# Scores of the next tile first in TensorE's step, their copy early in ScalarE's, and GpSimd's low parts of the weights one step later

## The reference, cut to what matters

```python
# B, H, S, D = 2, 8, 576, 64; N = 1152 tokens of 512
scores = (q @ k.T) / sqrt(D)                       # 576 x 576 for each of 16 heads
kth = np.partition(scores, -32, axis=-1)[..., -32] # the 32nd largest of each row
scores = np.where(scores >= kth, scores, -1e9)
attn = softmax(scores)                             # exp(s - max) / (sum + 1e-9)
x = (attn @ v)                                     # 1152 x 512 after the heads are joined
h = x @ w_in                                       # 512 -> 2048
x = (h * sigmoid(h)) @ w_out                       # 2048 -> 512
P = exp(x @ w_gate - max), then 8 rounds of dividing by row sums and column sums
out = sum over 8 experts e of P[:, e] * (relu(x @ w1[e]) @ w2[e])   # 512 -> 1024 -> 512
```

## Time and profile before

| | us |
|---|---|
| median of three runs | 1318.68 |
| lowest and highest | 1318.45, 1321.45 |
| the profiled execution, its own time | 1318.84 |
| its span, first to last instruction | 1317.0 |
| TensorE busy | 1266.2 (96%) |
| VectorE busy | 655.0 (50%) |
| ScalarE busy | 457.2 (35%) |
| GpSimd busy | 365.8 (28%) |

### The profile page before, as it was taken

One profiled execution on the slowest core, in us unless ns is written; L12 is line 12 of the kernel. 1 busy time (PEld: TensorE's weight loads), 2 busy tenths in 40 slices (PEclk: granted clock), 3 DMA queues, 4 the chain that ended last, 5 costly groups with the idle time before them and its releaser, 6 DMA issues.

```text
span 1317.0 us, 21366 instructions
## 1 busy us (share of the span) xinstructions
PE 1266.2 (96%) x8109; PEld 1121.8 (85%) x8109; DVE 655.0 (50%) x1557; ACT 457.2 (35%) x960; POOL 365.8 (28%) x319
## 2 busy tenths in 40 slices
PE   6888999999999999999999999999999999999999
PEld 5677787887787898898898898898898998998997
DVE  6889999999999326422222222222222222222222
ACT  3666766767667323021121121121120220220210
POOL 2665434434444322031131131130230230330300
PEclk9999999999999999999999999999999999999999
DMA  5863746636536543120120120120220210210001
GB/s 139 290 213 122 270 154 226 219 97 222 197 126 237 218 193 95 32 64 19 47 64 13 52 64 0 63 64 0 64 64 0 64 60 3 64 49 15 0 0 72
DMA packets 72929, 130.14 MB, mean 99 GB/s; under 512 B 42016, under 2 KB 42016, under 8 KB 63648
## 3 DMA queue, kind: packets, MB, share of 16 engines
q1 hardware_dynamic: 72864, 129.27, 28.9%
HBM read 110.12 MB, written 19.14 MB: 98 GB/s over the span
## 4 chain that ended last, share of the span: by engine, by line
PE 78%; DVE 12%; POOL 5%; ACT 3%; issue 2%; DMA 0%; SPq 0%; ACTq 0%
PE banks L408 24%; PE banks L410 24%; PE banks L409 24%; DVE stats L861 5%; DVE rest L872 4%; PE banks L476 2%; POOL probs L1108 2%; POOL wd_lo L1086 2%; PE banks L443 2%; POOL wu_lo L1086 1%; PE banks L452 1%; DVE g_f L926 1%; PE banks L469 1%; ACT scores L684 1%; ACT wu_hi L760 1%
## 5 line engine op out<-in xcount | busy, mean ns | idle before, releaser
L821 ACT ACTIVATE h_hi<-banks 128x384 fp32r<-128x384 f32 x192 | 94.4, 492 | 624.8 <-PE banks L410 624.8
L408 PE MATMUL banks<-x_lo,wu_hi 128*128 128x384 f32 x768 | 257.2, 335 | 0.0
L410 PE MATMUL banks<-x_hi,wu_hi 128*128 128x384 f32 x768 | 256.8, 334 | 0.0
L409 PE MATMUL banks<-x_hi,wu_lo 128*128 128x384 f32 x768 | 256.8, 334 | 0.0
L1086 POOL TENSOR_TENSOR wu_lo<-wu_raw,wu_hi 128x512 fp32r<-128x512 f32 x76 | 95.9, 1299 | 559.4 <-ACT wu_hi L760 552.2
L987 DVE SCALAR_TENSOR_TENSOR h_lo<-banks,h_hi 128x384 fp32r<-128x384 f32 x192 | 106.8, 557 | 281.7 <-ACT h_hi L821 281.7
L1029 DVE SCALAR_TENSOR_TENSOR y_acc<-banks,plan_e,y_acc 128x512 f32<-128x512 f32 x135 | 101.3, 751 | 272.3 <-PE banks L410 272.3
L408 PE MATMUL banks<-wd_lo,h_hi 128*128 128x512 f32 x576 | 227.9, 396 | 0.0
L410 PE MATMUL banks<-wd_hi,h_hi 128*128 128x512 f32 x576 | 227.8, 396 | 0.0
L409 PE MATMUL banks<-wd_hi,h_lo 128*128 128x512 f32 x576 | 227.8, 396 | 0.0
L861 DVE MAX8 stats<-rest 128x8 f32<-128x576 f32 x216 | 156.1, 750 | 0.7
(11 more groups left out here) (103 smaller groups left out, 1810.2 us busy)
## 6 DMA issues: line engine op xcount, KB each, us to landing
wu_raw<-in_moe_w_dram SPq DMA_DIRECT2D x32, 512.0 KB, 3.7
wd_raw<-in_moe_w_dram SPq DMA_DIRECT2D x32, 512.0 KB, 3.7
wu_hi<-kept_up_hi SPq DMA_DIRECT2D x14, 1024.0 KB, 5.5
wu_lo<-kept_up_lo SPq DMA_DIRECT2D x14, 1024.0 KB, 8.5
wd_hi<-kept_down_hi SPq DMA_DIRECT2D x14, 1024.0 KB, 6.1
wd_lo<-kept_down_lo SPq DMA_DIRECT2D x14, 1024.0 KB, 8.5
q_nat<-in_q_dram SPq DMA_DIRECT2D x64, 72.0 KB, 2.2
wu_raw<-in_moe_w_in_dram SPq DMA_DIRECT2D x8, 512.0 KB, 4.6
```

The source lines that it names most:

```text
L408: pe.matmul(to, a_hi, b_lo, start=first, stop=False)
L409: pe.matmul(to, a_lo, b_hi, start=False, stop=False)
L410: return pe.matmul(to, a_hi, b_hi, start=False, stop=last)
L821: act.activation(h_hi[:, f, CH * c:CH * (c + 1)], ps_up[:, at % UBANKS, 0:CH], ACT.Relu).then_inc(h_hi_done, 1)
```

## The change

On TensorE `scores_of(step + 1)` becomes the first thing of the step, ahead of the first slice and of `weigh_values`. On ScalarE `copy_scores(step + 1)` moves from behind `copy_output` to right behind `copy_pT`, ahead of `g_high`, the first slice's tanh and `exp_scores`. On GpSimd the low parts of the weight pieces of a step are formed in the next step, right behind `lower_scores`. SyncE's loads of the next unit move one step later with them.

```diff
@@ SyncE
-                if split_at(step - 1):
-                    stream, n = split_at(step - 1)
-                    load_split(stream, n + 1, 0)
                 if split_at(step - 2):
                     stream, n = split_at(step - 2)
+                    load_split(stream, n + 1, 0)
+                if split_at(step - 3):
+                    stream, n = split_at(step - 3)
                     load_split(stream, n + 1, 1)
                     if n < SLOTS:
                         keep_unit(stream, n)
@@
-            load_split("down", UQ + 1, 1)
+            for half in range(2):
+                load_split("down", UQ + 1, half)
@@ TensorE
             for step in STEPS:
+                if step + 1 < ALL:
+                    scores_of(step + 1)
                 silu_slice(slice_at(step, 0))
                 if step < NT + FIRST_SLICE:
                     keep_clock(ps_m[:, 1, 0:P], 4)
                 if 0 <= step - 3 < ALL:
                     weigh_values(step - 3)
-                if step + 1 < ALL:
-                    scores_of(step + 1)
@@ ScalarE
                 if 0 <= step - 3 < ALL:
                     copy_pT(step - 3)
+                if step + 1 < ALL:
+                    copy_scores(step + 1)
                 g_high(slice_at(step - 1, 0))
@@
-                if step + 1 < ALL:
-                    copy_scores(step + 1)
                 split_pieces(pieces_at(step, 0))
@@ GpSimd
                     lower_scores(step - 2)
+                if step <= ALL:
+                    split_pieces(pieces_at(step - 1, 0))
+                    split_pieces(pieces_at(step - 1, 1))
@@
-                if step < ALL:
-                    split_pieces(pieces_at(step, 0))
-                    split_pieces(pieces_at(step, 1))
```

## The result

The changed kernel takes 1326.49 us, the median of six runs (1325.42 to 1332.27), against 1319.27 for the kernel before in the same comparison. The ratio is 1.0059, interval 1.0040 to 1.0078: slower by 7 us. I had forecast 1316.4 and a range up to 1321.5.

What follows compares the result with a forecast made beforehand. It took a ring of GpSimd, lower_scores and ScalarE to bound steps 4 to 18, and TensorE and VectorE in turns steps 23 to 71. The terms -10.4 + 8.1 = -2.3 us gave 1316.5, by the median 1316.4; range 1309.5 to 1321.5.

Steps and rivals of the forecast that it cites:

- The ring of low parts: Tiles 4 to 18: GpSimd's low parts, lower_scores and ScalarE's high part wait on each other, 6.00 us a step.
- The gain by filled waits for the transposed tile: Steps without a first slice: scores fill TensorE's 0.78 us wait, so 0.69 us goes away behind the values.
- tiles 4 to 18, -10.4 forecast: With low parts a step later, steps fall from 6.00 us to VectorE's 5.24; 10.4 us gained, bounds 5 to 11.1.
- four filler matmuls about 0.5: Tiles 4 to 18: time in us put down for TensorE's filler between a head's scores and the values.
- my way through TensorE: Tiles 4 to 18, steps with head and values: copies, scores, filler, values, output copy; 5.2 to 5.4 us.
- I cost it at nothing: SyncE's loads one step later: they should land in time; if uncovered, up to 3.6 us, once or twice.
- I count none in the sum: Low-clock stretches from added TensorE waits: none counted, as ten earlier waits of 0.78 us came with one stretch.
- tiles 23 to 71, +8.1 forecast: Scores first: heads wait for ScalarE's copies, partly offset in steps without a first slice; sum 9.5, taken as 8.1 us.
- (b): Every head's step lengthens by the full stall, in both engines' stretches: 21 x 0.85 us; near 1324, chance 0.12.
- (c): TensorE's stretches: added waits lower the clock three more times, 1.9 us each; time 1322, chance 0.05.
- (d): First stage: ScalarE's way through TensorE replaces the ring at 5.6 us a step, gain 5; time 1322, chance 0.08.
- (a): The ring goes, VectorE bounds the steps and TensorE's added waits are hidden; near 1311 us, chance 0.30.

Runs made afterwards that it cites:

- e7: Changed kernel with scores behind the first slice, ahead of the values, and the second down unit's stores at SyncE's step 12: 1304.36 us, ratio 0.9886.
- e3: Changed kernel, but for tiles that begin a head the scores and their copy stay at their old places: 1308.48 us, ratio 0.9916.
- e1: Kernel before with only GpSimd's low parts and SyncE's loads one step later: 1314.25 us, ratio 0.9963.
- e11: Changed kernel with four small matmuls before each wait for a head's k and q, and the second down unit's stores at SyncE's step 12: 1326.48 us.
- e5: Changed kernel with the two stores of the second down unit at SyncE's step 12 instead of 10: 1326.43 us, ratio 1.0050.
- e10: Changed kernel with four small matmuls of the identity ahead of each wait for a head's k and q: 1327.92 us, ratio 1.0064.
- e4: Changed kernel with scores behind the first slice, ahead of the values, and their copy behind that slice's tanh: 1305.80 us, ratio 0.9896.
- e8: Changed kernel with ScalarE's copy of the scores back behind the copied output: 1324.54 us, ratio 1.0032.
- e12: Scores behind the first slice, second down unit's stores at step 12, and the head's transposes ahead of those of the probabilities: 1302.19 us, ratio 0.9875.
- e9: Changed kernel with the coming head's transposes ahead of those of the probabilities on TensorE: 1319.99 us, ratio 1.0000.

## Why the prediction was wrong

**Where the mechanism was right.** The ring of low parts was what bound tiles 4 to 18, and VectorE's 5.24 us a step is what lies below it: e7 reaches it exactly. The price of one wait, 1.01 us where k is copied too, was right to the digit. The gain by filled waits for the transposed tile is there, if smaller than forecast: e3, which keeps it, is 4.0 us below before in tiles 23 to 71 (1.5 of it the low clock that before happened to have at 286 us: 54.02 in that half, 52.51 with the same order in e1).

**The step that failed: tiles 4 to 18, -10.4 forecast, -4.3 measured.** One term in it was half its size, and three things stood at nothing.

- The term "four filler matmuls about 0.5" had no row behind it. The trace of the kernel before, from the first filler to the scores, has 1.01 us:

```profile
81.49 1.08 PE L563 MATMUL banks<-ident 128*128 128x128 f32 x8
82.50 0.76 PE L443 MATMUL banks<-kT,qT 64*128 64x288 f32 x4
```

  With it my way through TensorE is not 5.2 to 5.4 us but 5.7 to 5.9, above VectorE's 5.24 and above the 5.6 that I had set as the worst.
- "The steps between have a microsecond of slack, so I let VectorE's 5.24 hold." With the low clock and the jam away, scores first still costs 75.96 - 73.37 = 2.6 us (e11 against e7, with four fillers in the place of each wait): 2.0 at tiles 4 and 13, behind heads, and 0.6 at tile 11, where nothing waits for k and q. I had looked for the round back to ScalarE. The chain of after shows the other way to VectorE, the one through TensorE's spread of the row sums (L500), for which VectorE's scaling near the end of its step waits.
- SyncE's loads: "I cost it at nothing." I had checked whether the weights come in time. They do. What came late was a head's q. With the loads one step later the stores of two units are issued 4 us apart (63.5 and 67.3 us) instead of 10 (58.1 and 68.3 in the kernel before), stores and loads fill the DMA engines from 66 to 83 us, and the 72 KB of q behind them land in 4.7 us instead of 1.8 to 2.7 (the kernel before, e5, e7). e10 against e11, both without low clock there, gives 0.85 us, and the runs of e5 at equal clock about 1; e4 against e7 gives 2.5 with the low clock that the longer wait for q_nat brought. In the changed kernel it is part of tile 13's 9.35.
- The clock: "I count none in the sum." e10 against the changed kernel gives 2.8 us in this stage.

The last three, 2.6, 0.85 and 2.8 us, add up to 79.61 - 73.37 = 6.2 because they are the steps of one path, from the changed kernel to e10, e11 and e7. The sum is no check on them: in another order each could come out otherwise. I had named as a sign of being wrong that steps 4 to 18 stay above 5.5 us; they are at 5.69 on average. The gain at 5.6 a step was also summed wrongly: 83.93 - 14 x 5.6 is 5.5 and not 5.

**The mis-sized term: tiles 23 to 71, +8.1 forecast, +11.5 measured.** My own sum was 9.5, and I shaved it to 8.1 on grounds that no row carried. That is 1.4 of the 3.4 us. The rest is 0.3 to 0.5 us a half by ScalarE's early copy, which I had called free (e8); a gain behind the values of about 0.5 instead of 0.69 a half, after what the early copy costs there (e3 against before in halves without low clock: 50.34 to 50.85, 52.63 to 53.09), and one stretch of low clock gained at 212 us against one lost at 286. Another 0.5 us fell at step 22, which I had left out.

**The rivals.** (b), slower by the bare wait at every head, was the right direction for the stage from tile 23 on, at 0.77 a head instead of my 0.85, and I had given it 0.12. (c), the clock, was a real part, not a rest: in the changed kernel three stretches, in e5 seven, in e7, e11 and e12 none up to 430 us. Its place was not where I had it, though: the one stretch more than before lies in tiles 4 to 18, and in tiles 23 to 71 there is one as before. A stretch costs 1.4 to 1.5 us in a half of TensorE's stage, where I had said 1.9, and those from 28 and 86 us together 2.8 over tiles 4 to 18. That the throttled state is the default and activity releases it, as the Trainium skill's page "TensorE: Matmul & The Clock Gate" (Part 1, "What's actually happening") says, fits the direction of these runs. (d) had nearly the number, 5.6 us a step and 5 us gained, against 5.69 and 4.3. It didn't have the place: most steps run at 5.2 to 5.3, and three long ones make the mean. (a) was wrong: VectorE's being busy for 97% of the stage did not hide TensorE's waits, since the two take turns.

What stays open: how the causes in tiles 4 to 18 share a single step such as tile 13's, since no run had the jam without any wait for k and q and at full clock; and what, beyond a wait and its length, decides that the clock falls behind one wait and not behind the next.

## What to carry to other kernels

Don't move a producer and its consumer next to each other in the order of an engine that bounds the stage if another engine has to copy in between: the copy's whole latency, here 0.7 to 1.0 us with the hand-overs, is then in series at every such place, where one slice of other work hid it. When an order is changed, list for each moved wait what stood in front of it before, and try the nearest place that still has it in front: here scores behind the first slice instead of ahead of it made the difference between +7 and -13 us. Where queues shift too, look for what is small and urgent behind what is large, not only for the moved transfer itself. And read every term of the path that you say has slack from a row: the filler here was twice what I had put down.

## What the runs showed of the hardware that I had not expected

Waits of TensorE of 0.8 to 2.2 us were followed by some 3.4 us at 1.2 GHz, behind some of them and not behind others. Long waits did it far more often: in the profiles of the changed kernel, e5 and e9 there are 15 such stretches up to 430 us, and 14 of them begin within a wait of 1.5 to 2.2 us for a copied q or at most 1.7 us behind it. The other follows two waits of 0.70 and 0.79 us, 1.5 us apart; none follows a single wait of 0.49 or 0.79 for a copied q. Yet the kernel before has one 2.9 us behind a single wait of 0.78. Runs of the changed kernel spread over 6.9 us, with mean granted clocks from 0.992 (1332.27 us) to 0.997 (1325.42 us); with the waits filled the spread was 1.8 and 0.3 us. A 72 KB load took 4.7 us behind 4 MB of stores and some loads, at a DMA share of 1.04 over 17 us, and at most 2.4 us with half of the stores moved away (e5):

```profile
66.00:83.00 17.00, 16.21 (x171) 13.42 (x169) 16.50 (x49) 12.88 (x27) 11.84 (x10) 1.00 1.04 373
```
